# A recurrence, a feed-forward layer and an expert layer on one Trainium2 core: the opening's raw products, one diagonal and the order of the way back are moved

## What is computed

```python
def _attn_ref(r, k, v, w, u):            # r, k, v: (2, 8, 768, 48); w, u: (8, 48)
    for t in range(S):
        cur = np.einsum('bhd,bhe->bhde', u[None] * kt, vt)
        y[:, :, t] = np.einsum('bhd,bhde->bhe', rt, state + cur)
        state = w[None, :, :, None] * state + np.einsum('bhd,bhe->bhde', kt, vt)

x = y as 1536 rows of 384
h = x @ w_in;  g = where(h > 0, h, exp(min(h, 0)) - 1);  x2 = g @ w_out      # 384 -> 2048 -> 384
per row of x2: gate by softmax over 8 experts, the best one chosen,
out = gate * (max(x2 @ w1[e], 0) @ w2[e])                                   # 384 -> 1024 -> 384
```

## Time and profile before

| | |
|---|---|
| median of 3 runs | 416.25 us (415.97 to 416.66) |
| the profiled execution | 416.52 us |
| its span, first to last instruction | 414.7 us |
| PE busy | 406.5 us (98% of the span) |
| DVE, ACT, POOL busy | 242.7, 188.4, 231.8 us (59%, 45%, 56%) |

### The profile page before, as it was taken

How to read it: one execution, slowest core, us unless ns; L and a number is a source line. 1 busy time by engine, 2 the same in 40 slices (tenths; PEclk the granted TensorE clock), 3 DMA queues, 4 the chain that set the end, 5 groups by cost and what they waited for, 6 DMA issues and landing times.

```text
span 414.7 us, 9451 instructions
## 1 busy us (share of the span) xinstructions
PE 406.5 (98%) x3697; PEld 390.2 (94%) x3697; DVE 242.7 (59%) x576; ACT 188.4 (45%) x409; POOL 231.8 (56%) x239
## 2 busy tenths in 40 slices
PE   8999999999999999999999999999999999999994
PEld 8799799999999999999999999999999999999994
DVE  7787955375576547654754487775645546365421
ACT  4786543233433333333333555553645446464420
POOL 3789865467856685668234336075174461835531
PEclk9999999999999999999999999999999999999999
DMA  7999996204030403020018001827283844729000
GB/s 261 403 395 365 350 366 245 91 29 155 4 119 2 138 21 118 3 85 21 2 21 342 2 2 39 324 77 256 116 321 101 326 169 193 295 90 357 5 31 28
DMA packets 18650, 64.98 MB, mean 157 GB/s; under 512 B 2203, under 2 KB 11717, under 8 KB 16432
## 3 DMA queue, kind: packets, MB, share of 16 engines
q1 hardware_dynamic: 16816, 59.68, 39.5%
q0 software_dynamic: 1792, 4.73, 3.0%
HBM read 51.98 MB, written 13.21 MB: 157 GB/s over the span
## 4 chain that ended last, share of the span: by engine, by line
PE 89%; DVE 4%; DMA 3%; issue 1%; POOL 1%; ACT 1%; POOLq 0%; SPq 0%; DVEq 0%
PE bank L1362 26%; PE bank L1364 25%; PE bank L1363 25%; PE bank L1383 2%; DMA xrow<-slots 2%; PE bank L1412 1%; PE bank L1448 1%; PE bank L1452 1%; PE bank L1686 1%; PE bank L1441 1%; PE bank L1444 1%; PE bank L1539 1%; PE bank L1721 1%; PE bank L1722 1%; PE bank L1625 1%
## 5 line engine op out<-in xcount | busy, mean ns | idle before, releaser
L708 POOL TENSOR_TENSOR g_lo<-elu,g_hi 128x256 fp32r<-128x256 f32 x95 | 74.0, 780 | 86.3 <-ACT g_hi L875 85.7
L1362 PE MATMUL bank<-xt,wd_hi 128*128 128x256 f32 x285 | 80.5, 283 | 0.6 <-DVE elu L1190 0.6
L1364 PE MATMUL bank<-xt,wd_lo 128*128 128x256 f32 x285 | 80.4, 282 | 0.0
L1363 PE MATMUL bank<-xt,wd_hi 128*128 128x256 f32 x285 | 80.3, 282 | 0.0
L866 ACT ACTIVATE elu<-elu 128x256 f32<-128x256 f32 x96 | 40.1, 418 | 76.4 <-DVE elu L1182 75.9
L1362 PE MATMUL bank<-wd_hi,g_hi 128*128 128x392 f32 (+1 forms) x192 | 67.4, 351 | 0.0
L1364 PE MATMUL bank<-wd_hi,g_lo 128*128 128x392 f32 (+1 forms) x192 | 65.2, 340 | 0.0
L1363 PE MATMUL bank<-wd_lo,g_hi 128*128 128x392 f32 (+1 forms) x192 | 65.1, 339 | 0.0
L1190 DVE SCALAR_TENSOR_TENSOR elu<-elu,bank 128x256 f32<-128x256 f32 x96 | 40.3, 420 | 41.1 <-ACT elu L866 41.1
L875 ACT CAST g_hi<-elu 128x256 fp32r<-128x256 f32 x96 | 39.0, 406 | 44.0 <-DVE elu L1190 44.0
L1362 PEld LDWEIGHTS bank<-xt,wd_hi 128*128 128x128 f32 x285 | 53.9, 189 | 1.3 <-DVE elu L1190 1.1
(11 more groups left out here) (220 smaller groups left out, 945.1 us busy)
## 6 DMA issues: line engine op xcount, KB each, us to landing
we_raw<-wexp SPq DMA_DIRECT2D x8, 1536.0 KB, 7.9
wd_raw<-wexp SPq DMA_DIRECT2D x8, 1536.0 KB, 8.9
rkt<-rkt SPq DMA_DIRECT2D x12, 512.0 KB, 5.8
nat<-nat SPq DMA_DIRECT2D x9, 672.0 KB, 5.1
xrow<-slots SPq DMA_DIRECT2D x16, 193.0 KB, 7.4
wd_raw<-win SPq DMA_DIRECT2D x4, 768.0 KB, 9.3
wd_raw<-wout SPq DMA_DIRECT2D x4, 768.0 KB, 9.7
wo_tr<-wouttr SPq DMA_DIRECT2D x1, 3072.0 KB, 18.6
```

The source lines that it names most:

```text
L708: nc.gpsimd.tensor_tensor(g_lo[:, f % 4, :], elu[:, f % 2, :], g_hi[:, f % 4, :].bitcast(F32), ALU.subtract).then_inc(s_glo, 1)
L1362: mm(dst, w_hi, x_hi, start=start, stop=False)
L1363: mm(dst, w_hi, x_lo, start=False, stop=False)
L1364: return mm(dst, w_lo, x_hi, start=False, stop=stop)
```

## The change

The change touches the opening alone, and has five parts.

- Chunk 0's raw products are made by GpSimd, as soon as `rkt` of chunk 0 has landed, and no longer by VectorE. VectorE's `raw_pair(1)` waits until they are made.
- The odd heads' diagonal of chunk 0 is made by VectorE in one multiplication of the identity with the scalars, both read with a broadcast, and no longer by ScalarE.
- GpSimd makes chunk 1's diagonal before `natural_k1(0)`, not behind it. ScalarE makes `x_hi(0)` before its copy of the state.
- TensorE does `bonus_sums(1)` before `scores(0)`, and `back(0)` before `outer(0)`. In `back(1)` the part that needs only scores and v comes first, and the part with the state last; the wait for the state stands between them.
- The sums of the bonus are made 8 columns wide and no longer 64 from chunk 2 on. This function is called for chunks 0, 1 and 2.

```diff
+            pool.wait_ge(s_rkt[0], 16)
+            nc.gpsimd.tensor_tensor(rk_pair(0), rkt[0][:, 0, :, :], rkt[0][:, 1, :, :], ALU.mult).then_inc(s_prod, 1)
             diagonal(0)
+            diagonal(1)
             pool.wait_ge(s_k1, 2)
             natural_k1(0)
-            diagonal(1)
             natural_k1(1)
...
             nc.scalar.copy(pwn[:, :], ps_y[1][:, :]).then_inc(s_pwn, 1)
-            half_diagonal(0)
             bonus_copy(1)
             half_diagonal(1)
             w_in_hi(0)
+            x_hi(0)
             act.wait_ge(s_u, 1)
             nc.scalar.copy(z[1][:, :, :], u_bank(0).rearrange("p (h e) -> p h e", h=HP)).then_inc(s_z, 1)
-            x_hi(0)
...
-                if c < 2 and j == 1:
-                    dve.wait_ge(s_half, c + 1)
+                if c == 0 and j == 1:
+                    dve.wait_ge(s_half0, 1)
+                elif c == 1 and j == 1:
+                    dve.wait_ge(s_half, 1)
...
-            raw_pair(0)
             queries(0)
             keys(0)
+            dve.wait_ge(s_prod, 1)
             raw_pair(1)
             queries(1)
             keys(1)
+            dve.wait_ge(s_bon, 1)
+            dve.wait_ge(s_const, NPOOLC)
+            V.tensor_tensor(att[0][:, 1, :, :], bc(ident[:, :].unsqueeze(1), [128, HP, C]),
+                            bc(bon[0][:, :].rearrange("s (h j) -> s j h", j=2)[:, 1, :].unsqueeze(2), [128, HP, C]),
+                            ALU.mult).then_inc(s_half0, 1)
             mask(0, 0)
...
-                    wait_if(pe, s_z, c)
...
                 old = has_state(c)
-                if old:
+                state_first = old and c > 1
...
+                if not ends:
+                    pe.wait_ge(s_z, n_states(c))
+                    last = from_state()
                 last.then_inc(s_y, 1)
...
+                width = C // 4 if c < 2 else 4
...
-                    last = mm(bonus_bank(c)[:, hp, :, :], rk_pair(c)[:, hp, :], bc(u_pair[:, hp, :].unsqueeze(1), [128, C // 4, 2]),
+                    last = mm(bonus_bank(c)[:, hp, 0:width, :], rk_pair(c)[:, hp, :], bc(u_pair[:, hp, :].unsqueeze(1), [128, width, 2]),
                               start=True, stop=True)
...
+            bonus_sums(1)
             scores(0)
-            bonus_sums(1)
             scores(1)
+            back(0)
             outer(0)
-            back(0)
             back(1)
             outer(1)
```

More of the change, by code:

```diff
@@ L219, in build @@
         s_half = sem("half_diagonal_ready")
+        s_half0 = sem("half_diagonal0_by_dve")
         s_pre = pair("diagonal_ready")
@@ L1436, in back, with from_state @@
                 old = has_state(c)
-                if old:
+                state_first = old and c > 1
+                def from_state():
                     for hp in range(HP):
@@ L1440, in back @@
                             rows = slice(64 * j, 64 * j + 64)
-                            mm(dst(2 * j, hp), z[p][rows, hp, 0:MAIN], r1[p][rows, hp, :], start=True, stop=False,
-                               skip_group_check=True)
+                            mm(dst(2 * j, hp), z[p][rows, hp, 0:MAIN], r1[p][rows, hp, :], start=state_first,
+                               stop=not state_first, skip_group_check=True)
                     for hp in range(HP):
-                        mm(dst(1, hp), z[p][:, hp, MAIN:2 * MAIN], r1[p][:, hp, :], start=False, stop=False,
+                        end = mm(dst(1, hp), z[p][:, hp, MAIN:2 * MAIN], r1[p][:, hp, :], start=False,
+                                 stop=not state_first, skip_group_check=True)
+                    return end
+                if state_first:
+                    from_state()
+                ends = state_first or not old
+                for j in range(2):
+                    for hp in range(HP):
+                        mm(dst(2 * j, hp), v_cols(c, hp, j)[0], att[p][:, j, hp, :], start=not state_first, stop=ends,
                            skip_group_check=True)
@@ L1447, in back @@
                     for hp in range(HP):
[L1448 to L1452, removed]
+                        last = mm(dst(1, hp), v_cols(c, hp, j)[1], att[p][:, j, hp, :], start=False, stop=ends and j == 1,
                                   skip_group_check=True)
+                if not ends:
+                    pe.wait_ge(s_z, n_states(c))
+                    last = from_state()
                 last.then_inc(s_y, 1)
             def bonus_sums(c):
+                width = C // 4 if c < 2 else 4
                 pe.wait_ge(s_up, 16)
```

## The result

| | before | changed |
|---|---|---|
| median of 20 runs each | 415.94 us (415.54 to 416.66) | 416.63 us (416.12 to 417.24) |
| ratio | | 1.0017, 95% interval 1.0011 to 1.0023 |
| the profiled execution, its span | 416.52, 414.7 us | 416.65, 414.9 us |

The changed kernel is slower by 0.69 us. That is clear of the measurement's noise with 20 runs, and it is less than the 0.2% which the prediction counted as a change. The forecast was +1.3, and the likeliest case (slower by over 0.2%) did not come: the result, 0.17%, lies just inside the case of no change, and inside the range. The forecast of 417.5 stood 0.87 us too high, and 0.31 of that is its base: the median of the kernel before is 415.94 over 20 runs, not the 416.25 of the first three.

A forecast was written before the change was run, and what follows sets the result against it. TensorE was taken as the bound from fc1(0, 0) on, with VectorE setting its start. That start moving from 15.64 to 16.95 gave +1.3 us, narrow sums nothing, for a median of 417.5 us, range 415.8 to 418.3.

The forecast's parts named there:

- the likeliest case: Whole kernel: slower by over 0.2%, given a chance of 0.54; within 0.2% had 0.40, faster 0.06.
- GpSimd's product holds VectorE: Opening, near 4.8 us: GpSimd's raw product locks the shared port, so the tables' last step comes 1.10 us later.
- a second table instruction of 0.42 us: Sign of being wrong: VectorE's table instruction of 5.11 keeps 0.42 us instead of lasting 1.5.
- Its two rows for the lock: VectorE's product of 8.05 (1.13 us for 0.69, beside an affine_select) and low part of 18.91 (1.65 us), cited as lock evidence.
- What is queued behind it: Opening after the late tables: transposes 8.22, masks from 11.35, back(0) 12.8, back(1) 14.4, fc1(0, 0) 16.95, +1.3 us.
- Narrow sums: Chunk 2's bonus sums, eight matmul records from 64 columns to 8: 0.02 us, set to nothing; upper bound 0.9.
- One for one to the end: From fc1(0, 0) on TensorE is the bound, so any shift of its start passes wholly to the end.
- if the start is right and the end is not: Sign: if fc1(0, 0) starts as forecast but the end differs, TensorE as the bound has failed.
- The number to predict is the start of `fc1(0, 0)`, 15.64 us: Base of the sum: that start in the kernel before's profile, against which 16.95 was forecast, +1.3 us.
- The other order at the lock: Rival, chance 0.24: VectorE's new multiplication precedes GpSimd's diagonal(1), masks start 0.5 earlier; +0.8 us, 417.0.
- No lock at the start: Rival, chance 0.16: GpSimd's product does not hold VectorE, fc1(0, 0) starts at 15.3; -0.35 us, 415.9.
- The idle time simply goes: Rival, chance 0.06: VectorE's 0.72 us idle before chunk 1's masks vanishes, narrow sums give 0.2; -0.9 us, 415.3.

The follow-up runs named there:

- experiment 2: Kernel before with only chunk 0's raw products moved to GpSimd: +0.57 us (ratio 1.0015).
- experiment 4: Changed kernel with GpSimd's product waiting until the tables are made: +0.97 us against the kernel before (ratio 1.0022).
- experiment 5: Changed kernel with GpSimd's product replaced by two memsets, leaving out chunk 0's raw products: 416.54 us, 0.63 above the kernel before, one execution.
- experiment 7: Kernel before with five useless matmuls between outer(1) and fc1(0, 0), delaying that start by 0.93 us: time +1.00 us (ratio 1.0026).
- experiment 8: Kernel before with ten useless matmuls ahead of fc1(0, 0), delaying it by 2.05 us: time +2.33 us (ratio 1.0053), five runs.
- experiment 9: Kernel before, unchanged, run again for a second profile: +0.08 us (ratio 1.0003); fc1(0, 0) started at 16.33.
- experiment 10: Kernel before with chunk 1's features loaded ahead of u_pair, issued at 1.75 instead of 2.22: -0.02 us (ratio 1.0006).
- experiment 3: Changed kernel with chunk 0's product back on VectorE and its odd heads' diagonal back on ScalarE: +0.58 us against the kernel before (ratio 1.0017).
- experiment 6: Changed kernel with GpSimd's chunk 1 diagonal waiting for VectorE's odd diagonal of chunk 0: +0.50 us against the kernel before (ratio 1.0022).
- experiment 1: Changed kernel with chunk 0's raw products back on VectorE, all else as changed: +0.64 us against the kernel before (ratio 1.0017).
- experiment 12: Kernel before with chunk 1's features loaded ahead of u_pair and back(1)'s mask wait moved behind the state's part: -0.27 us (ratio 0.9993).

## Why the prediction was right in its rows and off in its size

- **GpSimd's product holds VectorE: right.** Forecast: the tables' last step 1.10 late; `pwk2` went from 5.76 to 6.89, 1.13. It was the first of the two table instructions that was held, not the second, which makes no difference. The prediction had named "a second table instruction of 0.42 us" as a sign of being wrong, and it took 0.41: that sign was badly chosen, since either of the two can be the one that is held. Of its two rows for the lock, the first has an affine_select with a single input from SBUF, not two as it says. Experiments 2, 4 and 5 show the cause of VectorE's delay: it goes with the product wherever the product falls, and vanishes when GpSimd does not read. The loss of the whole change does not hang on it alone: the product by itself costs 0.57, the orders by themselves 0.58, and all parts but the product 0.64.
- **What is queued behind it: right.** Transposes 8.22 forecast, 8.31 measured; VectorE's new multiplication 10.20 and 10.23; masks from 11.35 and 11.27; `back(0)` 12.8 and 12.66; `back(1)` 14.4 and 14.28; `fc1(0, 0)` 16.95 and 16.85. Only `bonus_sums(0)`, which was to stay at 6.48, came earlier, at 6.18; the transposes behind it waited for the tables all the same.
- **Narrow sums: right.** From 21.83 to 22.75 it is 0.92 us with 8 columns; the same sums took 21.53 - 20.62 = 0.91 with 64 in the kernel before. The formula by columns that the Trainium skill states for a lone matmul (TensorE: Matmul & The Clock Gate, "Back-to-back issue gap") does not show here; the same section has one row for 1 to 64 columns, by which nothing is saved, and the trace agrees with that.
- **One for one to the end: right as far as the intervals of experiments 7 and 8 tell.** By the prediction's own sign ("if the start is right and the end is not") it would have failed: from `fc1(0, 0)` to the end it is 399.1 us in the first profile and 398.1 in the changed kernel's. The two experiments say that a late start is not regained, and the rows below where this profile of the kernel before had lost time.
- **The term that was mis-sized is the base of the sum: "The number to predict is the start of `fc1(0, 0)`, 15.64 us".** I took one execution's opening for the kernel's. The features of chunk 1 had landed at 6.7 in it, and that wait does not appear in its rows. In three further profiles of the same opening the start is 15.89 to 16.33, two of them reckoned back from the added matmuls. So the term was not 16.95 - 15.64 = 1.3 but some 0.9 (16.85 less the mean of 15.97), and 0.69 in the medians. The change costs less on the median than against a lucky execution. That it asks for the load 0.5 us later explains some 0.2 of the 0.5 us by my estimate under experiment 9; no run shows this part by itself, and experiment 10, which took the wait away, showed no gain. The median of the runs was no warning here: the first profiled execution was 416.52 in all, above the median, with a loss of 0.4 us near 97 us and a wait of 0.25 at 385 in it that the changed kernel's profile does not have.
- **The rivals.** *The other order at the lock* was decided by 0.08 us (GpSimd asks at 10.15, VectorE at 10.23), as forecast; its price was not 0.5 but 0.2, because the scores hold the masks next. *No lock at the start* was priced at -0.35; experiment 5 is that case, and stands at +0.63 in one execution, since the load holds VectorE instead. *The idle time simply goes* did not occur: in experiment 3 it moved from chunk 1's masks to chunk 0's.

What is left of the difference between 0.88 and 0.69 is within what single profiles and these intervals can tell. The shift of 1.21 between the first profile and the changed kernel's shrinks in two places above all. Near 97 us TensorE loses 0.4 us within one group of matmuls, in the first profile

```profile
96.73 0.91 PE L1448 MATMUL bank<-att,nat 128*32 128x128 f32 x14
```

and not in the changed kernel's:

```profile
97.91 0.62 PE L1463 MATMUL bank<-att,nat 128*32 128x128 f32 x16
```

No semaphore releases it. It is there in experiments 6, 7, 8 and 9 as well, which are the whole of one group, and in none of the eight others. So it goes with the group in which an execution was timed and not with the kernel. The medians of the kernel before fit: 416.29 in that group, 415.86 and 415.91 in the other two, and 416.25 in the three runs on which the prediction was based, against 415.92 in the 17 others of its 20. The first profile and the changed kernel's therefore seem to come from two levels that lie 0.4 us apart, and the span of the one cannot be compared with that of the other. Experiments 1 to 4 and 6 to 9 ran on the same chip, so the chip is not what makes the difference; what does stays open.

The second place is the last expert's transposes, which wait for a load of gathered rows:

```profile
385.31 0.88 PE L1686 MATMUL bank<-ident,xrow 128*128 128x128 f32 x6 [0.25 <-DMA xrow<-slots]
```

They start 0.59 us behind the matmul in front of them in the first profile, and 0.18 in the changed kernel's, so 0.41 is lost. That load lands 8.9 to 9.5 us after its issue, and TensorE loses between 0 and 0.44 us there over the 14 profiles. In the kernel before alone it is 0.41 in one profile and 0.03 in the other, so it is chance of the execution.

## What to carry to other kernels

Before moving an operation to an engine that shares a port, write down which instruction of the other engine runs at that moment and what it reads: the move cost nearly the whole of the moved instruction there, here 1.13 us to save 0.60. And before a profile's start time is used as the base of a sum in the opening, ask of each load there how far its landing is from the moment it is asked for. Here it was 0.7 us (6.74 against 7.45), and the landing varied by 1.8 from profile to profile, so one profile was not enough. And before two profiles are compared to the end, ask whether they were taken together: the same kernel's median lay 0.4 us apart between groups.

## What the runs showed of the hardware that I had not expected

- One load of 512 KB, the second of that size, issued at 2.2 us with the same loads around it, landed 4.3 to 6.0 us later over twelve profiles. In the two of the unchanged kernel before it is 4.5 and 6.0.
- The same 26 warm-up records from 1.15 us on took between 4.75 us (experiment 6) and 5.92 us (experiments 2, 10 and 12), before anything in these kernels differs on TensorE. The unchanged kernel had 5.06 and 5.70. The first sums start at 6.46 to 6.48 behind the shorter ones where they need VectorE's product, and at 6.85 to 6.86 behind the longest, 0.4 us later.
- GpSimd's memsets ran beside VectorE's two-input instructions with no loss to VectorE (0.42 us apiece, as without them), while an affine_select with a single input from SBUF cost VectorE 0.44 us (1.13 for 0.69).
- A stall of 0.4 us within one group of matmuls, released by no semaphore, was in all four profiles of one group of timings and in the first profile, and in none of the nine others, whatever the kernel.
